# Two chained MLPs: a new order of three engines at the handover, and seven relayed waits in place of 21

## The chip, the core and the metric

The kernel runs on one core of a Trainium2 chip. The metric is the device time of a run in microseconds (us), the median of several runs. The engines that matter are TensorE (PE, matrix products), ScalarE (ACT) and VectorE (DVE), which read the products' results from PSUM and prepare the next operands in SBUF; GpSimd (POOL) does almost nothing, and SyncE (SP) issues the transfers. Each engine works through its own list of instructions strictly in the order in which the kernel's author wrote it. Semaphores are the only tie between the lists: an instruction waits until a count is reached, and everything behind it on its engine waits too.

## The reference

```
# q, k, v: 6016 tokens x 256 channels
qn, kn = q / norm over tokens, k / norm over tokens
a  = softmax(kn^T qn / tau)            # 256 x 256, over the channels
x1 = v @ a                             # 6016 x 256
h1 = x1 @ moe_w_in                     # 256 -> 2048
x2 = (h1 * cos(h1)) @ moe_w_out        # 2048 -> 256     first MLP
h2 = x2 @ moe2_w_in                    # 256 -> 2048
y  = (h2 * sigmoid(h2)) @ moe2_w_out   # 2048 -> 256     second MLP
```

## The kernel before

The first 60 us compute the softmax, which is then folded into the first MLP's input weights. After that come two passes over the tokens, one for each MLP. Tokens are cut into 12 tiles (`TILES`), tile 0 of 384 tokens and eleven of 512; a tile is worked on in halves of 192 or 256 columns. The 2048 hidden channels are cut into 4 steps a tile (`STEPS`). A step q therefore stands for one tile and one quarter of the hidden channels: steps 0 to 47 are the first MLP, steps 48 (`M1`) to 95 the second. Step 48 begins with tile 0 again, so the steps 48 to 51 are 192 columns wide.

A step's 2x2 block product is done in seven products in place of eight (a Strassen-Winograd form), with sums formed on ACT and DVE. Every number is split into a high and a low part, so each block takes three matmuls ("three passes"). In the code:

- `hidden(i, q)` is product i of the input side of step q, six matmuls (`xf_hi,h1w` in the first MLP, `xf_hi,h2w` in the second). It needs results of ACT and DVE: product 1 needs the PSUM bank pair of step q-2 free (`g_ps_ready`, `sil_ps_ready`), 6 and 2 need `s1`, 7 needs `s2`, 4 needs `s3`, 5 needs `c12` of step q-1, 3 needs `c22`.
- `output1(q, groups)` is the output side of the first MLP: eight groups of six matmuls (`g_hi,w1out`), always eight, of which group 0 waits for `lo_of_g(q)`.
- `output2(q, products)` is the output side of the second MLP: seven products (`g_hi,o2w`). Products 1, 2, 3 wait for `lo_s`, 5 and 7 for `lo_13`, 6 and 4 for `lo_24`. At step 48, products 5 and 6 also write PSUM banks that hold the first MLP's last result until ACT has moved it out (`move_x`, semaphore `x_moved`).
- On ACT (lines 469 to 594), `s1`, `s2`, `s3` copy products; `sine` and `hi_of_g` belong to the first MLP, `silu`, `silu_ps`, `hi_s`, `hi_13`, `hi_24` to the second; `hi_of_form(t)` splits the input of tile t.
- On DVE (lines 878 to 972), `c22`, `c12` form sums that `hidden` waits for; `gate`, `gate_ps`, `lo_of_g` belong to the first MLP; `t13`, `t2`, `t4`, `lo_s`, `lo_13`, `lo_24` to the second.

Inside an MLP the order within a step is always the same (`first_mlp(q)`, `second_mlp(q)`), and output runs three steps behind the hidden side in the first MLP (`output1(q - 3, ...)`) and two behind in the second. Around step 48 the order is written out by hand on each engine. There the first MLP's last three output steps (45, 46, 47) have to be worked off while the hidden side of steps 48, 49 and 50 begins.

A "relayed wait" sits in the middle of a product: `three_passes` issues its first matmul, and then the second one waits for `relay_done`, which POOL raises with a one-column memset (line 412) once `hidden(1, q)` is done. `RELAYED` (line 70) lists the steps q that have one. In the first MLP it stands in `output1(q - 3)`, group 1, in the second in `output2(q - 2)`, product 1; both come right behind `hidden(1, q)`. The data that the wait guards is not used by anyone: `relay` is read by nothing.

Of the kernel before, what the change touches and what calls it, by code (L numbers as in the profile page):

```python
# [27 lines left out]
def channel_attention_two_mlps(nc: bass.Bass, qk, v_tiles, tau, w_in1, w_out1, w_forms2, y_tiles):  # L28
# [21 lines left out]
    TILES = len(N)  # L50
    assert 2 * sum(N) == n_tokens and max(N) <= HALF
    STEPS = FC // 4
    M1 = TILES * STEPS
    ALL = 2 * M1
    LAST = ALL + 2

    def width(q):
        return N[q // STEPS % TILES]
# [8 lines left out]
        return 0 <= q < ALL  # L67


    RELAYED = [t * STEPS + 2 for t in range(2 * TILES) if t % TILES >= 1 + (t < TILES)]  # L70
    RELAY_TURN = {q: turn + 1 for turn, q in enumerate(RELAYED)}

    WP = 1024
# [10 lines left out]
    with ExitStack() as ctx:  # L84
# [203 lines left out]
        with nc.Block() as block:  # L288
# [126 lines left out]
            def _(act):  # L415
# [53 lines left out]
                def s1(q):  # L469
                    n = width(q)  # L470
                    act.wait_ge(p_done[1], q + 1)
                    if q < 2:
                        act.wait_ge(wu_slot7, q + 1)
                    if in1(q - 2):
                        act.wait_ge(g_ps_ready, q - 1)
                    if in2(q - 1):
                        act.wait_ge(sil_ps_ready, q - M1)
                    nc.scalar.activation(banks[:, c11_bank(q), :, 0:n], banks[:, c21_bank(q), :, 0:n],  # L478
                                         ACT.Copy).then_inc(s1_ready, 1)

                def s2(q):
                    n = width(q)
                    act.wait_ge(p_done[6], q + 1)
                    if q >= 1:
                        act.wait_ge(c12_ready, q)
                    nc.scalar.activation(s_part[:, 0, :, 0:n], banks[:, c21_bank(q), :, 0:n], ACT.Copy).then_inc(s2_ready, 1)  # L486

                def s3(q):
                    n = width(q)
                    act.wait_ge(p_done[7], q + 1)  # L490
                    if q >= 1:
                        act.wait_ge(c22_ready, q)
                    nc.scalar.activation(s_part[:, 1, :, 0:n], banks[:, c21_bank(q), :, 0:n], ACT.Copy).then_inc(s3_ready, 1)
# [30 lines left out]
                def hi_of_g(q):  # L524
                    n, b = width(q), q % 2
                    act.wait_ge(g_ready, q + 1)
                    act.wait_ge(g_ps_ready, q + 1)
                    if q >= 2:
                        act.wait_ge(out_done[1], q - 1)
                    else:  # L530
                        act.wait_ge(fold_ready, 2 * STEPS)
                    nc.scalar.activation(g_hi[:, 4 * b:4 * b + 4, :, 0:n], work[:, 4 * b:4 * b + 4, :, 0:n],
                                         ACT.Copy).then_inc(g_hi_ready, 1)

                def move_x(t, d):
                    n = N[t]
                    act.wait_ge(out_done[d], STEPS * (t + 1))
                    if t > 0:
                        act.wait_ge(x_stored, 16 * t)
                    nc.scalar.activation(xo[:, 2 * d:2 * d + 2, 0:n], banks[:, x_bank(t, d), :, 0:n],  # L540
                                         ACT.Copy, scale=TWO_PI).then_inc(x_moved, 1)

                def silu(q):
                    n, i = width(q), q - M1
                    act.wait_ge(c22_ready, q + 1)
                    act.wait_ge(c12_ready, q + 1)
                    if i > 0:
                        act.wait_ge(lo_s_ready, i)
                        act.wait_ge(t2_ready, i)
                    else:  # L550
                        act.wait_ge(g_lo_ready, M1 - 1)
                    nc.scalar.activation(work[:, 0:4:3, :, 0:n], h[:, q % 2, :, :, 0:n], ACT.Silu).then_inc(sil_ready, 1)  # L552

                def silu_ps(q):
                    n, i = width(q), q - M1
                    act.wait_ge(p_done[2], q + 1)
                    act.wait_ge(p_done[4], q + 1)
                    if i > 0:
                        act.wait_ge(lo_s_ready, i)
                        act.wait_ge(t4_ready, i)  # L560
                    else:
                        act.wait_ge(g_lo_ready, M1 - 1)
                    nc.scalar.activation(work[:, 1:3, :, 0:n], banks[:, q % 2:q % 2 + 2, :, 0:n],
                                         ACT.Silu).then_inc(sil_ps_ready, 1)
# [12 lines left out]
                def hi_13(q):  # L577
                    n, i = width(q), q - M1
                    act.wait_ge(t13_ready, i + 1)
                    if i > 0:  # L580
                        for o in (5, 7):
                            act.wait_ge(o_done[o], i)
                    else:
                        act.wait_ge(out_done[1], M1)
                    nc.scalar.activation(g_hi[:, 3:5, :, 0:n], work[:, 4:6, :, 0:n], ACT.Copy).then_inc(hi_13_ready, 1)
# [154 lines left out]
                sine(M1 - 1)  # L740
                silu_ps(M1)
                s1(M1 + 1)
                silu(M1)
                hi_of_g(M1 - 1)
                hi_s(M1)
                hi_of_form(TILES + 1)
                s2(M1 + 1)
                s3(M1 + 1)
                silu_ps(M1 + 1)
                s1(M1 + 2)  # L750
                hi_13(M1)
                hi_24(M1)
                silu(M1 + 1)
                s2(M1 + 2)
                hi_s(M1 + 1)
                move_x(TILES - 1, 0)
                move_x(TILES - 1, 1)
                hi_13(M1 + 1)
                s3(M1 + 2)
                for q in range(M1 + 3, LAST + 1):  # L760
# [3 lines left out]
            def _(dve):  # L764
# [453 lines left out]
                sums_of_form(TILES + 1)  # L1218
                phase(M1 - 1)
                lo_of_g(M1 - 2)  # L1220
                c22(M1)
                gate_ps(M1 - 1)
                c12(M1)
                gate(M1 - 1)
                lo_of_g(M1 - 1)
                t13(M1)
                lo_s(M1)
                t2(M1)
                c22(M1 + 1)
                t4(M1)  # L1230
                for q in range(M1 + 2, LAST + 1):
                    second_mlp(q)

# [1 line left out]
            def _(pe):  # L1235
# [284 lines left out]
                hidden(6, M1)  # L1520
                hidden(2, M1)
                hidden(5, M1)
                hidden(7, M1)
                output1(M1 - 3, (3, 4))
                hidden(4, M1)
                output1(M1 - 3, (5, 6, 7))
                hidden(3, M1)
                output1(M1 - 2, (0,))
                hidden(1, M1 + 1)
                output1(M1 - 2, (1, 2, 3, 4, 5, 6, 7))  # L1530
                hidden(6, M1 + 1)
                hidden(2, M1 + 1)
                hidden(5, M1 + 1)
                hidden(7, M1 + 1)
                hidden(4, M1 + 1)
                output1(M1 - 1, range(8))
                for q in range(M1 + 2, LAST):
                    second_mlp(q)


# [34 lines left out]
```

## Time and profile before

| | |
|---|---|
| median of 3 runs | 1046.9 us (1046.73 to 1046.99) |
| the profiled execution's own time | 1043.53 us |
| its span, first to last instruction | 1041.6 us |
| granted TensorE clock, mean | 0.997 |
| PE busy | 1019.6 us (98%) |
| DVE busy | 954.4 us (92%) |
| ACT busy | 806.4 us (77%) |

The span is 1.9 us shorter than the profiled execution's time, and that time is 3.4 us below the median of the runs that weren't profiled. A matmul's recorded duration is longer than the distance to the next one, since they are pipelined: what a matmul costs is the distance between two starts. A count (x...) in a view by windows also takes in the two or so matmuls that were still running when the window began.

### The profile page before, as it was taken

Reading aid. Unit: us, or ns where it says so; the run is one execution under the profiler, and the core shown is the slowest. Engines: PE = TensorE matmul, PEld = TensorE weight load, DVE = VectorE, ACT = ScalarE, POOL = GpSimd, SP = SyncE. Lnnn points to the kernel's source line nnn. Section 1 sums busy time; section 2 is a strip of 40 time slices with the busy share of each in tenths; the row PEclk is TensorE's granted clock in tenths of the full one; section 3 lists DMA queues with packets and bytes.
Section 4 is the critical chain, followed back from the end, with each engine's and each line's share of the span. In section 5 each row is a group of like instructions: output and inputs, shape, how many; then the busy total and the mean of one; then the engine's idle time right before and its main releaser. Section 6 shows DMA issues by size and latency. Waiting matters only on the chain. (4 is left out here: it accounts for less than half of the span.)

```text
span 1041.6 us, 21201 instructions
## 1 busy us (share of the span) xinstructions
PE 1019.6 (98%) x8718; PEld 1013.5 (97%) x8718; DVE 954.4 (92%) x1061; ACT 806.4 (77%) x875; POOL 2.9 (0%) x28
## 2 busy tenths in 40 slices
PE   7989999999999999999999899999999999999997
PEld 7979999999999999999999899999999999999997
DVE  7999989999999999998887389999999999999997
ACT  7779868788788788787777468877877878788775
POOL 0000000000000000000000000000000000000000
PEclk9999999999999999999999899999999999999999
DMA  8830110330331312304147211001001101101000
GB/s 286 289 97 6 36 37 21 112 132 21 112 112 42 112 68 82 116 22 163 36 162 274 100 42 37 4 38 42 20 23 42 41 2 42 42 2 41 22 22 21
DMA packets 18285, 76.03 MB, mean 73 GB/s; under 512 B 1808, under 2 KB 5904, under 8 KB 16144
## 3 DMA queue, kind: packets, MB, share of 16 engines
q1 hardware_dynamic: 18192, 74.72, 20.5%
q8 instruction: 67, 1.10, 0.4%
q14 instruction: 26, 0.21, 0.1%
HBM read 47.71 MB, written 27.00 MB: 72 GB/s over the span
## 5 line engine op out<-in xcount | busy, mean ns | idle before, releaser
L1241 PE MATMUL banks<-g_lo,w1out 128*128 128x256 f32 (+1 forms) x768 | 213.2, 278 | 0.0
L1242 PE MATMUL banks<-g_hi,w1out 128*128 128x256 f32 (+1 forms) x768 | 212.9, 277 | 0.0
L1238 PE MATMUL banks<-g_hi,w1out 128*128 128x256 f32 (+1 forms) x768 | 212.9, 277 | 0.0
L1238 PE MATMUL banks<-g_hi,o2w 128*128 128x256 f32 (+1 forms) x672 | 185.9, 277 | 3.8 <-ACT xo L540 1.5
L1238 PE MATMUL banks<-xf_hi,h1w 128*128 128x256 f32 (+1 forms) x672 | 186.8, 278 | 2.9 <-ACT banks L478 2.0
L1238 PE MATMUL banks<-xf_hi,h2w 128*128 128x256 f32 (+1 forms) x672 | 186.4, 277 | 1.9 <-ACT s_part L486 1.3
L1242 PE MATMUL banks<-xf_hi,h2w 128*128 128x256 f32 (+1 forms) x672 | 186.2, 277 | 0.0
L1241 PE MATMUL banks<-xf_lo,h2w 128*128 128x256 f32 (+1 forms) x672 | 186.2, 277 | 0.0
L1241 PE MATMUL banks<-g_lo,o2w 128*128 128x256 f32 (+1 forms) x672 | 185.9, 277 | 0.0
L1241 PE MATMUL banks<-xf_lo,h1w 128*128 128x256 f32 (+1 forms) x672 | 185.8, 276 | 0.0
L1242 PE MATMUL banks<-xf_hi,h1w 128*128 128x256 f32 (+1 forms) x672 | 185.8, 276 | 0.0
L1242 PE MATMUL banks<-g_hi,o2w 128*128 128x256 f32 (+1 forms) x672 | 185.7, 276 | 0.0
L1241 PEld LDWEIGHTS banks<-g_lo,w1out 128*128 128x128 f32 x768 | 145.3, 189 | 0.0
L1238 PEld LDWEIGHTS banks<-g_hi,w1out 128*128 128x128 f32 x768 | 145.1, 189 | 0.0
L1242 PEld LDWEIGHTS banks<-g_hi,w1out 128*128 128x128 f32 x768 | 145.1, 189 | 0.0
L1238 PEld LDWEIGHTS banks<-g_hi,o2w 128*128 128x128 f32 x672 | 126.6, 188 | 4.5 <-issue 1.7
L1238 PEld LDWEIGHTS banks<-xf_hi,h1w 128*128 128x128 f32 x672 | 126.4, 188 | 4.3 <-ACT banks L478 2.6
L1238 PEld LDWEIGHTS banks<-xf_hi,h2w 128*128 128x128 f32 x672 | 127.0, 189 | 2.2 <-ACT s_part L486 1.5
L1241 PEld LDWEIGHTS banks<-xf_lo,h2w 128*128 128x128 f32 x672 | 127.1, 189 | 0.0
L1242 PEld LDWEIGHTS banks<-xf_hi,h2w 128*128 128x128 f32 x672 | 127.1, 189 | 0.0
L1241 PEld LDWEIGHTS banks<-xf_lo,h1w 128*128 128x128 f32 x672 | 126.7, 188 | 0.1
L1242 PEld LDWEIGHTS banks<-g_hi,o2w 128*128 128x128 f32 x672 | 126.5, 188 | 0.0
(123 smaller groups left out, 2322.0 us busy)
## 6 DMA issues: line engine op xcount, KB each, us to landing
w_scr<-w_split SPq DMA_DIRECT2D x8, 1792.0 KB, 7.5
qk_raw<-qk SPq DMA_DIRECT2D x23, 512.0 KB, 4.5
h2w<-w_scr SPq DMA_DIRECT2D x4, 1792.0 KB, 8.0
o2w<-w_scr SPq DMA_DIRECT2D x4, 1792.0 KB, 8.1
form<-v_tiles SPq DMA_DIRECT2D x11, 512.0 KB, 3.5
x_scr<-xo SPq DMA_DIRECT2D x11, 512.0 KB, 2.6
form<-x_scr SPq DMA_DIRECT2D x11, 512.0 KB, 4.1
y_tiles<-xo SPq DMA_DIRECT2D x11, 512.0 KB, 5.0
```

The lines of the kernel that those rows point to most:

```text
L1238: nc.tensor.matmul(out, w_hi, m_hi, start=start, stop=False, skip_group_check=True)
L1241: nc.tensor.matmul(out, w_hi, m_lo, start=False, stop=False, skip_group_check=True)
L1242: return nc.tensor.matmul(out, w_lo, m_hi, start=False, stop=stop, skip_group_check=True)
```

## The change

Nothing is added to or taken from what is computed. Two things differ.

First, the order of the hand-written handover. PE lists the same products in another order, and now writes step 50 out by hand as well. ACT and DVE swap neighbours. On SyncE the list is the same.

Second, `RELAYED` holds 7 steps in place of 21. Before: step 2 of every tile from tile 2 on in the first MLP (q = 10, 14, ... 46) and from tile 1 on in the second (q = 54, 58, ... 94). Now: q = 7, 10, 14, 22 in the first MLP and q = 54, 58, 66 in the second.

```diff
-    RELAYED = [t * STEPS + 2 for t in range(2 * TILES) if t % TILES >= 1 + (t < TILES)]
+    RELAYED = [STEPS + 3] + [t * STEPS + 2 for t in (2, 3, 5, TILES + 1, TILES + 2, TILES + 4)]
...
@@ scalar engine @@
                 s1(M1 + 1)
+                hi_of_g(M1 - 1)
                 silu(M1)
-                hi_of_g(M1 - 1)
+                s2(M1 + 1)
+                s3(M1 + 1)
                 hi_s(M1)
                 hi_of_form(TILES + 1)
-                s2(M1 + 1)
-                s3(M1 + 1)
                 silu_ps(M1 + 1)
+                hi_13(M1)
                 s1(M1 + 2)
-                hi_13(M1)
+                move_x(TILES - 1, 0)
                 hi_24(M1)
                 silu(M1 + 1)
+                move_x(TILES - 1, 1)
                 s2(M1 + 2)
                 hi_s(M1 + 1)
-                move_x(TILES - 1, 0)
-                move_x(TILES - 1, 1)
@@ vector engine @@
+                gate_ps(M1 - 1)
                 c22(M1)
-                gate_ps(M1 - 1)
+                gate(M1 - 1)
                 c12(M1)
-                gate(M1 - 1)
                 lo_of_g(M1 - 1)
                 t13(M1)
+                t2(M1)
                 lo_s(M1)
-                t2(M1)
+                t4(M1)
                 c22(M1 + 1)
-                t4(M1)
@@ tensor engine @@
                 hidden(5, M1)
+                output1(M1 - 3, (3,))
                 hidden(7, M1)
-                output1(M1 - 3, (3, 4))
+                output1(M1 - 3, (4, 5))
                 hidden(4, M1)
-                output1(M1 - 3, (5, 6, 7))
+                output1(M1 - 3, (6, 7))
+                output1(M1 - 2, (0, 1))
+                hidden(1, M1 + 1)
+                output1(M1 - 2, (2,))
                 hidden(3, M1)
-                output1(M1 - 2, (0,))
-                hidden(1, M1 + 1)
-                output1(M1 - 2, (1, 2, 3, 4, 5, 6, 7))
+                output1(M1 - 2, (3,))
                 hidden(6, M1 + 1)
+                output1(M1 - 2, (4, 5, 6))
+                hidden(7, M1 + 1)
+                hidden(5, M1 + 1)
                 hidden(2, M1 + 1)
-                hidden(5, M1 + 1)
-                hidden(7, M1 + 1)
+                output1(M1 - 2, (7,))
+                output1(M1 - 1, (0,))
                 hidden(4, M1 + 1)
-                output1(M1 - 1, range(8))
-                for q in range(M1 + 2, LAST):
+                output1(M1 - 1, (1, 2, 3, 4, 5, 6, 7))
+                hidden(1, M1 + 2)
+                output2(M1, (3,))
+                hidden(3, M1 + 1)
+                output2(M1, (1,))
+                hidden(6, M1 + 2)
+                output2(M1, (2, 7))
+                hidden(5, M1 + 2)
+                output2(M1, (5, 4))
+                hidden(7, M1 + 2)
+                output2(M1, (6,))
+                hidden(2, M1 + 2)
+                hidden(4, M1 + 2)
+                for q in range(M1 + 3, LAST):
                     second_mlp(q)
```

ACT's list in the first half of the handover, before the change. L478 is `s1`, L552 `silu`, L532 `hi_of_g`, L575 `hi_s`, L438 `hi_of_form`, L486 `s2`, L493 `s3`, L563 `silu_ps`; the names in brackets are semaphores that the instruction waits for.

```order
L478 ACTIVATE banks<-banks 128x2x192 [waits sil_ps_ready,g_ps_ready,p1_done]
L552 ACTIVATE work<-h 128x2x2x192 [waits g_lo_ready,c12_ready,c22_ready]
L532 ACTIVATE g_hi<-work 128x2048 [waits out_done_1,g_ps_ready,g_ready]
L575 ACTIVATE g_hi<-work 128x6x192 [waits out_done_1,sil_ps_ready,sil_ready]
L438 ACTIVATE xf_hi<-form 128x1792 [waits p3_done,form_sum]
L486 ACTIVATE s_part<-banks 128x2x192 [waits c12_ready,p6_done]
L493 ACTIVATE s_part<-banks 128x2x192 [waits c22_ready,p7_done]
L563 ACTIVATE work<-banks 128x4x192 [waits lo_s_ready,t4_ready,p4_done,p2_done]
```

The same stretch now:

```order
L478 ACTIVATE banks<-banks 128x2x192 [waits sil_ps_ready,g_ps_ready,p1_done]
L532 ACTIVATE g_hi<-work 128x2048 [waits out_done_1,g_ps_ready,g_ready]
L552 ACTIVATE work<-h 128x2x2x192 [waits g_lo_ready,c12_ready,c22_ready]
L486 ACTIVATE s_part<-banks 128x2x192 [waits c12_ready,p6_done]
L493 ACTIVATE s_part<-banks 128x2x192 [waits c22_ready,p7_done]
L575 ACTIVATE g_hi<-work 128x6x192 [waits out_done_1,sil_ps_ready,sil_ready]
L438 ACTIVATE xf_hi<-form 128x1792 [waits p3_done,form_sum]
L563 ACTIVATE work<-banks 128x4x192 [waits lo_s_ready,t4_ready,p4_done,p2_done]
```

`s2` and `s3` of step 49 have moved ahead of `hi_s(48)` and `hi_of_form(13)`, and `hi_of_g(47)` ahead of `silu(48)`.

ACT's list in the second half, from `s1(50)` to `hi_13(49)`, before the change. L585 is `hi_13`, L594 `hi_24`, L540 `move_x`.

```order
L478 ACTIVATE banks<-banks 128x2x192 [waits sil_ps_ready,p1_done]
L585 ACTIVATE g_hi<-work 128x4x192 [waits out_done_1,t13_ready]
L594 ACTIVATE g_hi<-work 128x4x192 [waits t4_ready,t2_ready]
L552 ACTIVATE work<-h 128x2x2x192 [waits lo_s_ready,t2_ready,c12_ready,c22_ready]
L486 ACTIVATE s_part<-banks 128x2x192 [waits c12_ready,p6_done]
L575 ACTIVATE g_hi<-work 128x6x192 [waits o2_done,o1_done,o3_done,sil_ps_ready,sil_ready]
L540 ACTIVATE xo<-banks 128x512 [waits x_stored,out_done_0]
L540 ACTIVATE xo<-banks 128x512 [waits x_stored,out_done_1]
L585 ACTIVATE g_hi<-work 128x4x192 [waits o7_done,o5_done,t13_ready]
```

And now:

```order
L585 ACTIVATE g_hi<-work 128x4x192 [waits out_done_1,t13_ready]
L478 ACTIVATE banks<-banks 128x2x192 [waits sil_ps_ready,p1_done]
L540 ACTIVATE xo<-banks 128x512 [waits x_stored,out_done_0]
L594 ACTIVATE g_hi<-work 128x4x192 [waits t4_ready,t2_ready]
L552 ACTIVATE work<-h 128x2x2x192 [waits lo_s_ready,t2_ready,c12_ready,c22_ready]
L540 ACTIVATE xo<-banks 128x512 [waits x_stored,out_done_1]
L486 ACTIVATE s_part<-banks 128x2x192 [waits c12_ready,p6_done]
L575 ACTIVATE g_hi<-work 128x6x192 [waits o2_done,o1_done,o3_done,sil_ps_ready,sil_ready]
L585 ACTIVATE g_hi<-work 128x4x192 [waits o7_done,o5_done,t13_ready]
```

`hi_13(48)` has moved ahead of `s1(50)`, and the two `move_x` ahead of `hi_24(48)` and `s2(50)`.

## Rows read from the trace of the kernel before

**Rows 1.** The page, busy time of each engine.

```profile
PE 1019.6 (98%) x8718; PEld 1013.5 (97%) x8718; DVE 954.4 (92%) x1061; ACT 806.4 (77%) x875; POOL 2.9 (0%) x28
```

**Rows 2.** Windows: stretch, length, busy us (count) of each engine, granted clock, DMA.

```profile
556.58:595.24 38.66, 34.25 (x266) 33.60 (x265) 19.64 (x21) 19.55 (x23) 0.00 (x0) 0.91 0.51 201
573.80:577.20 3.40, 3.40 (x18) 3.40 (x18) 0.69 (x2) 0.81 (x1) 0.00 (x0) 0.50 0.25 105
590.90:594.20 3.30, 3.30 (x18) 3.30 (x17) 1.14 (x3) 0.95 (x2) 0.00 (x0) 0.50 0.02 5
595.30:605.90 10.60, 10.60 (x97) 10.60 (x97) 7.86 (x9) 6.80 (x10) 0.00 (x0) 1.00 0.31 100
133.50:165.30 31.80, 31.80 (x273) 31.80 (x272) 27.42 (x29) 23.64 (x23) 0.00 (x0) 1.00 0.10 30
165.50:206.00 40.50, 40.50 (x359) 40.50 (x358) 38.72 (x38) 32.89 (x32) 0.00 (x0) 1.00 0.24 85
288.00:550.00 262.00, 262.00 (x2311) 262.00 (x2311) 244.40 (x226) 210.18 (x206) 0.62 (x7) 1.00 0.25 91
740.00:1007.00 267.00, 267.00 (x2355) 267.00 (x2355) 256.15 (x306) 213.08 (x239) 0.69 (x7) 1.00 0.09 27
```

**Rows 3.** Timeline of PE, handover: start, duration, instruction, [idle before <- releaser].

```profile
571.94 0.36 PE L1238 MATMUL banks<-xf_hi,h2w 128*128 128x192 f32 x1 [1.32 <-ACT s_part L486]
...
573.43 0.36 PE L1238 MATMUL banks<-xf_hi,h2w 128*128 128x192 f32 x1 [0.58 <-ACT s_part L493]
...
585.74 0.36 PE L1238 MATMUL banks<-g_hi,o2w 128*128 128x192 f32 x1 [0.97 <-DVE g_lo L965]
...
589.54 0.33 PE L1238 MATMUL banks<-g_hi,o2w 128*128 128x192 f32 x1 [1.54 <-ACT xo L540]
```

**Rows 4.** Timeline of ACT, handover.

```profile
557.99 1.92 ACT L521 ACTIVATE work<-work 128x2048 f32<-128x2048 f32 x1
560.16 1.28 ACT L563 ACT_TABLE_LOAD   x1 [0.24 <-DVE g_lo L927]
561.45 0.81 ACT L563 ACTIVATE work<-banks 128x768 f32<-128x768 f32 x1
...
564.09 0.84 ACT L552 ACTIVATE work<-h 128x768 f32<-128x768 f32 x1
564.83 1.91 ACT L532 ACTIVATE g_hi<-work 128x2048 fp32r<-128x2048 f32 x1
568.76 1.17 ACT L575 ACTIVATE g_hi<-work 128x1152 fp32r<-128x1152 f32 x1 [2.03 <-PE banks L1242]
569.83 1.68 ACT L438 ACTIVATE xf_hi<-form 128x1792 fp32r<-128x1792 f32 x1
571.41 0.47 ACT L486 ACTIVATE s_part<-banks 128x384 f32<-128x384 f32 x1
572.89 0.49 ACT L493 ACTIVATE s_part<-banks 128x384 f32<-128x384 f32 x1 [1.00 <-PE banks L1242]
...
583.47 0.47 ACT L478 ACTIVATE banks<-banks 128x384 f32<-128x384 f32 x1 [7.86 <-PE banks L1242]
583.86 0.84 ACT L585 ACTIVATE g_hi<-work 128x768 fp32r<-128x768 f32 x1
...
588.80 1.08 ACT L540 ACTIVATE xo<-banks 128x512 f32<-128x512 f32 x2
```

**Rows 5.** Timeline of DVE, handover.

```profile
560.44 1.21 DVE L921 TENSOR_TENSOR work<-work,banks 128x1024 f32<-128x1024 f32 x1
...
584.72 0.96 DVE L965 TENSOR_TENSOR g_lo<-work,g_hi 128x768 fp32r<-128x768 f32 x1 [10.23 <-ACT g_hi L585]
```

**Rows 6.** Timeline of POOL: the first relay memset.

```profile
165.40 0.10 POOL L412 MEMSET relay<- 128x1 f32 x1 [163.94 <-PE banks L1242]
```

**Rows 7.** Timeline of PE at the second relayed wait.

```profile
206.48 0.31 PE L1241 MATMUL banks<-g_lo,w1out 128*128 128x256 f32 x1
206.62 0.28 PE L1242 MATMUL banks<-g_hi,w1out 128*128 128x256 f32 x1
```

## The prediction

> **What bounds the kernel now.** I read the page first. PE is busy for 98% of the span, DVE for 92%, ACT for 77% [rows 1]. So two questions are left: where does PE stand still, and how far apart do its matmuls start where it doesn't? The view of waits and the timeline of PE answer the first. Between the start-up and the last output step, which the change doesn't touch, PE has one cluster of stalls, in the handover. There are four, each with its releaser [rows 3]:
>
> - 571.94, product 7 of step 49, released by `s2(49)`. ACT started `s2` at 571.41 because `hi_s(48)` and `hi_of_form(13)` stood ahead of it [rows 4]; its own input, product 6, had ended near 569.1 (PE ran dry near 570.5, two products of 0.67 us later).
> - 573.43, product 4 of step 49, released by `s3(49)`: product 4 stood right behind product 7, and `s3` (0.49 us) had no room between them.
> - 585.74, output product 7 of step 48, released by `lo_13(48)` on DVE, which had idled 10.23 us for `hi_13(48)` [rows 5]. That was queued on ACT behind `s1(50)`, which waited 7.86 us for PE [rows 4].
> - 589.54, output product 5 of step 48, released by the first `move_x` at 588.80, which was queued behind `hi_s(49)`.
>
> The view by windows shows that the granted clock fell to 0.50, that is 1.2 of 2.4 GHz, in two stretches, each just behind two such stalls (from 573.80 and from 590.90) [rows 2]. Elsewhere in the handover it was 1.00.
>
> The same view answers the second question. Leaving out the matmuls still running at a window's start, about 2.4, the 256-column ones start 31.80/270.6 = 0.1175 us apart from 133.5 to 165.3, and 40.50/356.5 = 0.1136 us apart from 165.5 to 206 [rows 2]. It is the same code at two paces, at full clock in both. What lies between is the first relayed wait [rows 6]. The faster pace then holds: 262/2308.5 = 0.1135 from 288 to 550, and 267/2352.5 = 0.1135 from 740 to 1007. So a relayed wait puts PE into the quicker pace, and once there it stays. Why, the trace doesn't show.
>
> **Part 1, the handover.** Both kernels hold the same products between 556.58 (behind hidden product 5 of step 48) and the end of product 4 of step 50, at 595.24 before. That is 38.66 us with 266 - 2 = 264 matmuls: 21 output groups of the first MLP, 126 matmuls of 256 columns, and 138 of 192. Without stalls and at full clock, at the slower pace, which the change doesn't alter here, they take 126 x 0.1175 = 14.8 us, plus 138 x 10.60/94.6 = 0.112, 15.5 us (the window from 595.30) [rows 2]. Together 30.3 us, so 8.4 us can go. The other way round: four idle times of 1.32 + 0.58 + 0.97 + 1.54 = 4.41 us, each 0.16 us short of what it costs (a 0.27 us matmul's successor starts after 0.11), make 5.05 us. The low clock costs 3.40 - 16 x 0.1135 = 1.6 and 3.30 - 16 x 0.112 = 1.5 us. That is 8.2 us, with the edges of the slow stretches left out. I take 8.4.
>
> Whether it goes depends on what is late next. I laid the new lists side by side, with 0.67 us for a product of 192 columns, 0.705 for a group of 256, and the durations of rows 4 and 5. A PE result is usable some 0.16 us after its product's slot ends. "Ready" is when the operand is there, "wanted" when PE reaches the product:
>
> - `gate_ps(47)` for product 1 of step 49: product 7 of step 48 now ends at 557.96, so `s3(48)` ends 558.6, `sine(47)` (1.92) at 560.5, `gate_ps` (1.21, now first on DVE) at 561.7. Wanted 562.9.
> - `s1(49)` for product 6: product 1 ends 563.5, ready 564.2, wanted 565.6.
> - `s2(49)` for product 7: ACT does `hi_of_g(47)` 564.1 to 566.0, `silu(48)` to 566.7 (its `c12(48)` is there at 565.7), `s2` to 567.1. Wanted 568.4.
> - `s3(49)` for product 4: product 7 ends 569.1, ready 569.7, wanted 571.8. Three products and two groups stand between now.
> - `lo_s(48)` for output product 3: output step 46 ends 571.1, `hi_s` (1.17) 572.4, `lo_s` about 573.8, wanted 578.1.
> - `lo_13(48)`: output step 47 ends 577.4, `hi_13` 577.6 to 578.4, `lo_13` (0.96) to 579.4, wanted 581.4.
> - `s1(50)`, now behind `hi_13`: ready 578.8, wanted 580.1.
> - both `move_x`: ready about 579.4 and 581.5, wanted 582.8 and 584.8.
> - `s2(50)`: ready 582.0, wanted 584.1. `s3(50)`, behind `hi_s(49)` and `hi_13(49)`: product 7 ends 584.8, ready 585.4, wanted 586.2. This is the tightest, 0.8 us, and is the spacing that `second_mlp` has in every step.
>
> What the moves delay: `hi_s(48)` and `hi_of_form(13)` (1.68 us) run 3 to 4 us later on ACT's clock, and behind them stands `silu_ps(49)`, done by 575.2 and needed for `s1(50)` at 578. DVE's `c12(48)` waits for product 3 of step 48 until 565.0, with only `lo_of_g(47)` queued behind it, which ends at 568.3 and is wanted at 571.1. SP's list is the same; its weight load for step 50 waits for the end of output step 46 and starts 2.6 us later, some 20 us before that step's output. ACT's table load (1.28 us) stays one load, ahead of `silu_ps(48)`. I charge nothing for any of these: the slack above covers them. If one cover fails it costs what is short, bounded above by the longest stall of before, 1.7 us, and 1.7 more if the clock falls; below nothing, since no product becomes shorter.
>
> **Part 2, the earlier relayed wait.** A step of the first MLP is 90 matmuls. The wait at q = 7 stands three steps ahead of the one at q = 10, that is 3 x 90 x 0.1175 = 31.7 us before 165.4, at 133.7. From there everything is 256 columns wide. If it does what the one at 165.4 did, 270 matmuls gain 0.1175 - 0.1135 = 0.004 us each: 1.1 us. Bounds: nothing, if the pace doesn't turn there (the wait at q = 10 is still in the list), and 1.2 by the step lengths. At the quicker pace DVE must keep up: it is busy for 38.72 of 40.50 us in the following tile, where weight work comes on top, and PE has no stall there; here it has 27.42 of 31.80 [rows 2]. So no charge. I take 1.1, since the one example seen, in the same place of a step, worked.
>
> **Part 3, 14 relayed waits fewer.** In the quick pace such a wait costs the distance 206.62 - 206.48 = 0.14 less 0.1135 [rows 7]: 0.03 us. 14 fewer give 0.4 us. Bounds: 0 and 0.5. What goes with them is the insurance. From q = 22 to the handover, 260 us, and from q = 66 to the end, some 290 us, nothing resets the pace. Against a slip speaks that in the windows of 262 and 267 us, waits every 40 us never found a slow pace to repair: the mean 0.1135 leaves no room for even one slow tile.
>
> The TensorE page of the Trainium skill (TensorE: Matmul & The Clock Gate, "Back-to-back issue gap") gives an isolated full-clock gap of N/2.4 + 2.5 ns, which is 109 ns at 256 columns as an estimate, and knows no second pace. By it the wait at q = 7 would bring nothing, which is rival 1 below, and the sum would be 8.8 us. The trace differs: 0.1175 and 0.1135 us at full clock.
>
> **Sum.** 8.4 + 1.1 + 0.4 = 9.9 us. The profiled execution's 1043.5 us becomes 1033.6. It stands 3.4 us below the median of the runs, and nothing here depends on that difference, so 1046.9 - 9.9 = 1037.0 us.
>
> **Rivals.**
>
> 1. *The wait at q = 7 doesn't turn the pace.* Only one turn is seen after a slow stretch of the first MLP, so a turn may need a position that happens to fit. Then 1.1 us are missing, the extra wait costs 0.03: 1038.1 us.
> 2. *A new wait takes the place of an old one in the handover.* My lists are hand-timed to a few tenths, and the slack is 0.8 to 1.4 us at five places. A stall of about 1 us costs 1 us, and with a second one close by the clock falls again (1.7): 1038.0 to 1039.7 us. Against it: the two pairs of stalls before came from waits of 2 us and more.
> 3. *The clock falls without the stalls,* for instance from the change of widths. Then 3.3 us stay: 1040.3 us. Against it: both falls stand right behind two stalls, and none elsewhere.
> 4. *Slower: the pace slips where no relayed wait is left.* At 0.1175 a matmul, an unguarded stretch loses 3.5%, 9 us from q = 22 on and 10 from q = 66 on. Eating up the 9.9 us takes 280 of the 550 unguarded us, that is a slip at the beginning of one stretch and an early one in the other. Both at once: 1037.0 + 19 = 1056 us. For it speaks that a slow pace did come about by itself: the stretch from 133.5 on follows the narrow tile 0. Against it: after 165 us no slip anywhere in uniform work.
>
> **How the numbers follow.** The forecast has a chance of 62%, rival 1 of 13%, rival 2 of 13%, rival 3 of 4%. A slip as in rival 4 has 8%, of which 3 end slower than before. The forecast's own range is 1036.2 to 1037.8 (the remainders of the terms: +-0.4 on the handover, 0.1 on each of the others, 0.2 between sessions). To hold 8 in 10 it has to take in rivals 1 and 2: 1036.1 to 1039.7. About 0.2% is what a measurement can tell here; faster by more than that 0.95, within it 0.02, slower 0.03.
>
> **What the profile would show.** Right: no PE idle time over 0.3 us between 550 and 590, granted clock 1.00 there, product 4 of step 50 ending near 586.9 - 1.1 - 0.2 = 585.6; `s2(49)` ahead of `hi_s(48)` on ACT; POOL memsets at about 133.7 and then 164.3, with 0.1135 us between matmuls in between; 0.1135 from 290 to 540 and from 730 to the end; PE's total gap 9.9 us smaller. Wrong: a memset at 133.7 with 0.1175 behind it (rival 1), a wait on `s3`, `s1` or `lo_13` in the handover (rival 2), a window at 0.50 (rival 3), or 0.1175 anywhere behind q = 22 outside the narrow tile (rival 4).

## The result, and the profile after

The changed kernel took 1034.86 us (median of 4 runs, 1033.86 to 1036.12) beside 1046.82 us for the kernel before (4 runs, 1046.03 to 1046.99). That is 12.0 us less, a ratio of 0.9888 with a 95% interval of 0.9871 to 0.9905. The predicted 1037.0 us was 2.1 us too high, and its range, from 1036.1, missed the median. The two profiled executions differ by less: 1043.53 and 1034.61 us, 8.9 us. The start-up (up to the first full-width `hidden` product) takes 1.6 us off that difference: it ends at 103.5 us in the trace before and at 105.0 in this one, although both kernels are the same up to there.

Page part 1 of the kernel after; it answers [rows 1].

```profile
span 1032.7 us, 21187 instructions
PE 1015.8 (98%) x8718; PEld 1010.7 (98%) x8718; DVE 954.4 (92%) x1061; ACT 806.6 (78%) x875; POOL 1.5 (0%) x14
```

The same windows, where they have a counterpart [rows 2]: the handover, the stretch between the memsets of q = 7 and q = 10, and one long stretch without a relayed wait in each MLP.

```profile
556.00:586.00 30.00, 30.00 (x267) 30.00 (x267) 19.37 (x22) 20.30 (x24) 0.00 (x0) 1.00 0.67 268
135.30:165.70 30.40, 30.40 (x270) 30.40 (x269) 27.09 (x29) 23.52 (x23) 0.00 (x0) 1.00 0.11 32
290.00:550.00 260.00, 260.00 (x2296) 260.00 (x2296) 242.53 (x223) 208.62 (x204) 0.00 (x0) 1.00 0.25 92
732.00:1000.00 268.00, 268.00 (x2367) 268.00 (x2366) 257.12 (x310) 214.33 (x240) 0.00 (x0) 1.00 0.09 27
```

PE is busy through the whole handover, at a granted clock of 1.00; before, 34.25 of 38.66 us at 0.91. Less the 2.4 matmuls that were running at a window's start, the other three windows give 0.1136, 0.1134 and 0.1133 us a matmul: the quick pace begins at q = 7, and it holds for 260 and 268 us without a wait.

The timeline of ACT in the handover, whose rows answer [rows 4].

```profile
558.66 1.91 ACT L521 ACTIVATE work<-work 128x2048 f32<-128x2048 f32 x1
...
566.68 0.48 ACT L486 ACTIVATE s_part<-banks 128x384 f32<-128x384 f32 x1
569.26 0.49 ACT L493 ACTIVATE s_part<-banks 128x384 f32<-128x384 f32 x1 [2.10 <-PE banks L1242]
571.41 1.17 ACT L575 ACTIVATE g_hi<-work 128x1152 fp32r<-128x1152 f32 x1 [1.66 <-PE banks L1242]
572.48 1.69 ACT L438 ACTIVATE xf_hi<-form 128x1792 fp32r<-128x1792 f32 x1
...
577.53 0.84 ACT L585 ACTIVATE g_hi<-work 128x768 fp32r<-128x768 f32 x1 [2.16 <-PE banks L1242]
578.28 0.47 ACT L478 ACTIVATE banks<-banks 128x384 f32<-128x384 f32 x1
578.69 0.58 ACT L540 ACTIVATE xo<-banks 128x512 f32<-128x512 f32 x1
...
584.82 0.49 ACT L493 ACTIVATE s_part<-banks 128x384 f32<-128x384 f32 x1 [0.45 <-PE banks L1242]
```

`s2(49)` ends at 567.2 (forecast 567.1), `s3(49)` at 569.8 (569.7), `hi_13(48)` at 578.4 (578.4), `s3(50)` at 585.3 (585.4). The times can be compared as they stand, since both traces reach step 48 at almost the same time (552.53 and 552.65 us): the longer start-up happens to cancel what was gained behind q = 7. On DVE, `lo_13(48)` follows at once, and DVE idles 3.50 us ahead of it where it idled 10.23 [rows 5]:

```profile
578.40 0.96 DVE L965 TENSOR_TENSOR g_lo<-work,g_hi 128x768 fp32r<-128x768 f32 x1 [3.50 <-ACT g_hi L585]
```

### The profile page after: what moved, and what is told of

Same layout as the page of the kernel before. It is cut to its first block, busy times and chain, and to the rows that moved or that the text cites. A ratio compares the mean times of both kernels' runs of the same rounds, so it can differ in the third digit from the quotient of the medians.

```text
span 1032.7 us, 21187 instructions
## 1 busy us (share of the span) xinstructions
PE 1015.8 (98%) x8718; PEld 1010.7 (98%) x8718; DVE 954.4 (92%) x1061; ACT 806.6 (78%) x875; POOL 1.5 (0%) x14
## 4 chain that ended last, share of the span: by engine, by line
PE 96%; DVE 1%; ACT 1%; issue 1%; DMA 0%; DVEq 0%; ACTq 0%
PE banks L1238 31%; PE banks L1241 30%; PE banks L1242 30%; PE banks L1254 2%; PE banks L1256 2%; PE banks L1258 1%; PE banks L1264 0%; DMA qk_raw<-qk 0%; ACT w1in_hi L431 0%; ACT g_hi L575 0%; ACT work L521 0%; DVE wr L856 0%; DVE qk_lo L767 0%; DVE h L893 0%; DVE g_lo L965 0%
## 5 line engine op out<-in xcount | busy, mean ns | idle before, releaser
L1238 PEld LDWEIGHTS banks<-xf_hi,h1w 128*128 128x128 f32 x672 | 127.2, 189 | 4.2 <-ACT banks L478 2.6
L1242 PEld LDWEIGHTS banks<-xf_hi,h1w 128*128 128x128 f32 x672 | 127.1, 189 | 0.0
L1242 PEld LDWEIGHTS banks<-xf_hi,h2w 128*128 128x128 f32 x672 | 126.4, 188 | 0.0
```

The costliest lines, as they stand in the source:

```text
L1238: nc.tensor.matmul(out, w_hi, m_hi, start=start, stop=False, skip_group_check=True)
L1242: return nc.tensor.matmul(out, w_lo, m_hi, start=False, stop=stop, skip_group_check=True)
```

## The experiments

All times are medians, and each group is compared with runs of the kernel before on its own chip.

**The kernel before, six traces.** The first question was what the first trace had less of than the first median. Five more executions of the unchanged file were traced.

> The kernel before, word for word, for a second trace and for the spread of its runs. Its trace behind the prediction was an execution of 1043.5 us, 3.4 us below the median of its other runs. Theory A (the missing 2 us come from stretches at the lower granted clock that this one trace happened to have few of): this execution takes 1045 to 1047 us, and its trace shows more time at granted clock 0.50 than the 3.4 + 3.3 us of the first, in the handover or in the start-up between 60 and 90 us. Theory B (the pace of TensorE differs from run to run): the trace shows 0.1175 us between matmuls in uniform work somewhere behind 165 us. Theory C (an offset outside the span): span plus 1.9 us no longer gives the time.

> The kernel before once more, for a third trace. Theory B (whether a relayed wait turns the pace is chance): the spacing from 166 to 207 us is 0.1175 or 0.1135, and the segment between the first and the second memset is 42.4 or 40.8 us, nothing between. Theory A (the low clock varies): the segment from step 48 to the memset of step 54 is 72.0 us with one fall less, or 73.6 us. The time of this execution differs from the first trace's by the sum of such pieces and by the start-up's (103.4 to 105.8 us up to the first full-width product).

> The kernel before, a fourth trace, to find out what its executions above 1046 us hold. If the time comes out above 1045.8: the start-up up to the first full-width product takes 105 us or more (in place of 103.4 to 104.2), or the wait at q = 10 fails to turn the pace (segment 42.4 in place of 40.8 us), or both; the handover segment is 72.0 or 73.6 us. If it comes out below: the same pieces add up to less.

> The kernel before, a fifth trace, with the same expectation: the time is the sum of start-up (103.4 to 105.8 us), the segment up to q = 14 (with 1.6 us for each tile in which the wait failed) and the handover (72.0 or 73.6 us), within 0.2 us.

> The kernel before, a sixth trace, with the same expectation. Together the six say how often each piece occurs, and so whether the 3.4 us between the first trace and the first median can be made of them.

Measured, with segments read from the starts of PE and POOL instructions (us). "Start-up" ends where the first full-width `hidden` product starts; "tile 2" is the distance from the memset of q = 10 to that of q = 14; "handover" goes from step 48's first matmul to the memset of q = 54.

| trace | time | start-up | tile 2 | handover |
|---|---|---|---|---|
| before, first | 1043.5 | 103.5 | 40.8 | 73.6 |
| e1 | 1044.4 | 104.2 | 42.4 | 72.0 |
| e8 | 1044.3 | 104.0 | 40.8 | 73.7 |
| e10 | 1044.2 | 103.9 | 42.4 | 72.2 |
| e11 | 1046.6 | 106.5 | 42.4 | 72.0 |
| e12 | 1043.5 | 103.1 | 42.4 | 72.1 |
| after, first | 1034.6 | 105.0 | 40.8 | 64.9 |
| after, e4 | 1036.5 | 105.8 | 40.8 | 64.9 |
| after, e14 | 1035.7 | 105.0 | 40.8 | 64.9 |

Theory B's sign, the slow pace behind 165 us, is there in four of the five new traces. Theory A did not come as written: e1 took 1044.4 us, below its 1045, with as much time at the low clock as the first trace (one stretch of 3.4 us in the start-up and one in the handover, in place of two in the handover). But the low clock does vary in both places. What lies outside the span is 1.9 to 2.0 us in all (theory C is out). By the medians, e1 (1044.66 us, 10 runs, ratio 1.0003) and e8 (1044.48, 10 runs, 1.0001) are the same as before. The trace above 1046 us is e11. Its windows in the start-up, one inside the handover, and then the two tiles behind q = 10 and q = 14:

```profile
72.00:82.00 10.00, 9.53 (x54) 9.44 (x55) 7.06 (x14) 4.79 (x11) 0.00 (x0) 0.66 0.01 2
579.00:583.00 4.00, 4.00 (x23) 4.00 (x22) 0.09 (x1) 0.81 (x1) 0.00 (x0) 0.57 0.07 29
134.00:168.00 34.00, 34.00 (x291) 34.00 (x290) 29.31 (x31) 24.44 (x24) 0.00 (x0) 1.00 0.09 29
168.50:210.50 42.00, 42.00 (x359) 42.00 (x358) 38.77 (x38) 32.80 (x32) 0.00 (x0) 1.00 0.23 82
211.00:291.00 80.00, 80.00 (x708) 80.00 (x707) 76.55 (x73) 65.30 (x64) 0.10 (x1) 1.00 0.24 86
```

And its relay memsets:

```profile
168.35 0.10 POOL L412 MEMSET relay<- 128x1 f32 x1 [166.88 <-PE banks L1242]
210.76 0.10 POOL L412 MEMSET relay<- 128x1 f32 x1 [42.31 <-PE banks L1242]
251.60 0.10 POOL L412 MEMSET relay<- 128x1 f32 x1 [40.75 <-PE banks L1242]
```

At 168.35 the relayed wait did nothing: 42.00/356.6 = 0.1178 us a matmul for another tile. The next, at 210.76, turned the pace (80.00/705.6 = 0.1134). The granted clock was low in the start-up for some 30 matmuls in a row, 6.4 us, against some 15 in e1, e8 and e10 and none in the first trace and e12. So the start-up ends at 103.1 to 106.5 us, later than e11's own expectation allowed, and the changed kernel's varies as well (105.0 to 105.8). Over all 17 traces it ends at 103.1 to 103.5 us without low clock, at 103.6 to 105.0 with one such stretch of 15 matmuls and at 105.8 to 106.5 with two: the low clock goes with most of the spread, not with all of it. The handover holds one low stretch in four traces and two in the others. The trace of 1046.6 us is 3.06 us above the first: 3.01 from the start-up, 1.57 from tile 2, less 1.62 in the handover.

Over all these comparisons, 14 of 52 runs of before were above 1046 us (and 5 of 20 in e1 and e8), and its medians on four further chips were 1044.6 to 1045.3 us. The first median of 1046.9 us, on which the prediction was built, stands for 4 runs of 4 above 1046 us.

The traces show one more thing. Whether the first relayed wait turns the pace goes with something that happens some 9 us ahead of q = 7, in code that is the same in all the kernels here. Between two narrow output groups of tile 0 stand 24 full-width matmuls. Here are the first and the twenty-first of them, in the first trace of the kernel after (above) and in e4 (below):

```profile
125.92 0.30 PE L1238 MATMUL banks<-xf_hi,h1w 128*128 128x256 f32 x1
128.30 0.28 PE L1242 MATMUL banks<-xf_hi,h1w 128*128 128x256 f32 x1
```

```profile
126.68 0.30 PE L1238 MATMUL banks<-xf_hi,h1w 128*128 128x256 f32 x1
129.00 0.28 PE L1242 MATMUL banks<-xf_hi,h1w 128*128 128x256 f32 x1
```

The distance is 2.38 us in the one and 2.31 in the other, and in the 17 traces of this document it is always one of these two. Where it was 2.38, the first relayed wait turned the pace, 8 times of 8 (the first trace before, e8, e2, after, e3, e13, e9, e7; e6 has no wait). Where it was 2.31, the first wait did nothing, 8 times of 8 (e1, e10, e11, e12, e4, e14, e5, e15), and the second wait turned the pace every time. Before the wait, all 17 ran at the slow pace again. Why the two cases arise, and how they reach the wait, no run shows.

**The two halves of the change.** `RELAYED` of before in the file of after (e2), and of after in the file of before (e3), beside the changed kernel (e4).

```diff
# e2: after, with
+    RELAYED = [t * STEPS + 2 for t in range(2 * TILES) if t % TILES >= 1 + (t < TILES)]
# e3: before, with
+    RELAYED = [STEPS + 3] + [t * STEPS + 2 for t in (2, 3, 5, TILES + 1, TILES + 2, TILES + 4)]
```

> The new order of the handover with the 21 relayed waits of before. The prediction's own terms: 8.4 us faster than before. Theory A: 10 to 11 us faster, since the typical run of before loses more in the handover than its trace showed. Theory B: 8.4 to 9 us faster. In the trace no stall and no low clock between 550 and 590 us under all of them.

> The old order of the handover with the seven relayed waits of after. The prediction's own terms: 1.1 + 0.4 = 1.5 us faster than before. Theory A: the same 1.5 us, as the waits have nothing to do with the handover's stalls. Theory B: 3 to 4 us faster. The four stalls of the handover stay under all of them.

> The changed kernel again, beside the two halves: 11 to 12.5 us faster than before. If the two halves are independent, the gain of the order and the gain of the waits sum to this within 0.7 us. Its handover shows no low clock; what still varies between its runs lies in the start-up before 100 us (theory A).

Measured against 1044.82 us (19 runs, 1043.97 to 1047.91): the order alone 1035.87 (ratio 0.9919, 0.9902 to 0.9935), 9.0 us faster; the waits alone 1043.17 (0.998, 0.9968 to 0.9992), 1.7 us faster; both 1035.51 (0.9911, 0.9894 to 0.9927), 9.3 us faster, not 11 or more. The halves sum to 10.6, 1.3 us more than the whole and more than the 0.7 expected; the spread of single runs (e3: 1039.8 to 1045.5) leaves it open whether that is a difference. In e2's trace the handover has no stall and no low clock. In e3's all four stalls are there, as expected, with one low stretch, behind the first pair:

```profile
573.20:576.50 3.30, 3.30 (x18) 3.30 (x17) 0.03 (x1) 0.81 (x1) 0.00 (x0) 0.50 0.06 26
```

The stretch from 290 to 550 us in e2, with six waits, has three matmuls less than the kernel after in the same 260 us:

```profile
290.00:550.00 260.00, 260.00 (x2293) 260.00 (x2293) 242.32 (x224) 208.10 (x204) 0.59 (x6) 1.00 0.26 92
```

Three matmuls are 0.3 us, 0.05 us a wait.

**No waits, and a wait in every step.**

```diff
# e6: after, with
+    RELAYED = []
# e7: after, with
+    RELAYED = list(range(STEPS + 3, M1)) + list(range(M1 + STEPS + 2, ALL))
```

> The changed kernel without any relayed wait. If only such a wait turns TensorE to the quicker pace, all uniform work from 134 us on runs at 0.1175 us a matmul: 3450 matmuls up to the handover and 3600 behind it, each 0.004 us dearer, is 28 us, so 26 to 30 us slower than the changed kernel. Rival (the pace turns by itself sooner or later, as in the narrow tile of the handover): less than 10 us slower. Rival (the waits only cost): 0.3 us faster than the changed kernel.

> The changed kernel with a relayed wait in every step, 83 in place of 7. At the 0.03 us of the prediction the 76 more cost 2.3 us; at the 0.045 us that the segments of the traces with 21 and 7 waits show, 3.4 us. Against this stands a turn to the quick pace at step 8 or 9 at the latest where q = 7 misses it, worth up to 1.2 us. So 1.5 to 3.5 us slower than the changed kernel. In the trace the spacing is 0.1135 plus one longer distance a step.

Without waits 1049.84 us (three runs of 4 at 1049.7 to 1050.0, one at 1066.0); before on the same chip 1044.59. The changed kernel didn't run on that chip; by its times and gains on the others this is 14 to 15 us slower than it, half of what was expected, except in one run. The windows of the trace say why:

```profile
135.00:165.00 30.00, 30.00 (x257) 30.00 (x256) 25.59 (x27) 22.73 (x22) 0.00 (x0) 1.00 0.11 32
290.00:550.00 260.00, 260.00 (x2210) 260.00 (x2209) 235.12 (x218) 199.94 (x196) 0.00 (x0) 1.00 0.24 86
640.00:1000.00 360.00, 360.00 (x3179) 360.00 (x3178) 346.48 (x412) 288.38 (x322) 0.00 (x0) 1.00 0.09 29
```

The whole first MLP ran at 260/2207.6 = 0.1178 us, and behind the narrow tile of the handover the second MLP ran at 0.1133 with no wait at all. In this trace the pace changed across the narrow tile of the handover, and uniform work kept what it had. The run of 1066 us would be one with the slow pace in both MLPs: 3600 matmuls at 0.0044 us more are 16 us (it took 16.2 us more than the median), and its granted clock, 0.998, was no lower than that of the others. It was not traced, so this is not shown.

A wait in every step: 1037.36 us, ratio 0.994 (0.9923 to 0.9957). Its memsets in the first MLP:

```profile
143.70 0.10 POOL L412 MEMSET relay<- 128x1 f32 x1 [10.15 <-PE banks L1242]
153.95 0.10 POOL L412 MEMSET relay<- 128x1 f32 x1 [10.15 <-PE banks L1242]
```

A step is 10.25 us with its wait, so four steps are 41.0 us. A tile with one wait is 40.84 us, so three more waits add 0.16, again 0.05 us each. The kernel is 7.2 us faster than before on its chip, 2 to 3 us less than the changed kernel is on the others, within the 1.5 to 3.5 expected.

**Which list does the work.** e5 keeps the new lists of ACT and DVE and the seven waits, and puts back TensorE's old handover. e13 keeps TensorE's new handover and puts back the second half of ACT's list.

```diff
# e5: after, TensorE's hand-written steps from hidden(5, M1) on as in before
# e13: after, scalar engine
-                hi_13(M1)
                 s1(M1 + 2)
-                move_x(TILES - 1, 0)
+                hi_13(M1)
                 hi_24(M1)
                 silu(M1 + 1)
-                move_x(TILES - 1, 1)
                 s2(M1 + 2)
                 hi_s(M1 + 1)
+                move_x(TILES - 1, 0)
+                move_x(TILES - 1, 1)
```

> The new lists of ScalarE and VectorE and the seven waits, but TensorE's handover in the order of before. If the stalls came from what stood ahead of s2(49), hi_13(48) and move_x on ScalarE, three of the four stalls go with these lists alone, and only the wait of product 4 of step 49 for s3(49) stays (0.74 us beyond the pace), because product 7 stands right ahead of it. A single short stall: if the clock falls only after two stalls close together, it stays at 1.00 and the kernel is 0.7 to 1 us behind the changed one. Rival: one stall is enough for a clock fall, then 2.3 to 2.6 us behind. Rival: TensorE's own order is what cures them, then 5 us or more behind.

> The changed kernel with ScalarE's second half as before: hi_13(48) behind s1(50), both move_x behind hi_s(49). TensorE's new order puts three more products between output step 47 and output product 7 of step 48, so lo_13 should still be in time (ready 580.6, wanted 581.4). move_x would now wait for hi_s(49), which waits for output product 2: ready near 583.7, wanted 582.8. So one stall of about 1 us at output product 5, a granted clock of 1.00, and 0.8 to 1.3 us slower than the changed kernel. Rival: the clock falls too, 2.4 to 3 us slower. Rival: the moves in this half weren't needed, the same time.

e5: 1036.71 us against 1044.59, ratio 0.9932 (0.9915 to 0.9948), 7.9 us faster. Three of the four stalls are gone, and the one that stays is the expected one, a wait for `s3(49)`; the window over the handover has no low clock.

```profile
572.21 0.36 PE L1238 MATMUL banks<-xf_hi,h2w 128*128 128x192 f32 x1 [0.58 <-ACT s_part L493]
```

```profile
560.00:600.00 40.00, 39.35 (x344) 38.98 (x343) 25.18 (x31) 23.67 (x31) 0.00 (x0) 1.00 0.49 184
```

Its handover segment is 66.3 us against 64.9 with TensorE's new order and 72.0 to 73.7 before. So of the 7.1 to 8.8 us that the handover gives, ACT's and DVE's lists alone bring all but 1.4, where 0.7 to 1 was expected. The stall is 0.74 of that. The trace has the rest in two pieces. A shorter hold-up, which shows as only 0.07 us of idle time, stands ahead of this matmul, which starts 0.35 us behind the one before it:

```profile
561.71 0.36 PE L1238 MATMUL banks<-xf_hi,h2w 128*128 128x192 f32 x1
```

With the slower matmuls beside it, it costs about 0.35 us. And the two long runs of full-width output groups go at the slow pace (42 matmuls from 563.84 at 0.1184 us and 48 from 572.97 at 0.1182), where the changed kernel takes 0.1146 for the 42 from 572.46: 90 x 0.0037, about 0.33 us.

The reverse, TensorE's new order with ACT's whole old list, was not tried: `s2(49)` would stand behind `hi_s(48)`, which waits for output step 46 (group 7), which TensorE's new order puts behind product 7 of step 49, which waits for `s2(49)`, so it would deadlock.

e13: 1035.65 us, ratio 0.9909 (0.9887 to 0.9931), beside 1034.73 for the changed kernel on the same chip. One stall, for `move_x`, and none for `lo_13`, as expected; no low clock.

```profile
583.03 0.33 PE L1238 MATMUL banks<-g_hi,o2w 128*128 128x192 f32 x1 [1.02 <-ACT xo L540]
```

```profile
560.00:600.00 40.00, 38.98 (x347) 38.84 (x346) 26.06 (x32) 24.52 (x32) 0.00 (x0) 1.00 0.48 180
```

The segment is 66.1 us: 1.2 us for moving two copies forward. In these two traces single stalls of 0.74 and 1.2 us left the clock at 1.00, and each low stretch of before followed a pair of stalls within 4 us. That is no proof that a single stall is safe: of the 14 pairs in the seven traces with the old lists, 9 were followed by a low stretch and 5 were not, and each single stall was traced once.

**Waits close together, and many runs of both.**

```diff
# e9, e15: after, with
+    RELAYED = [STEPS + 3, STEPS + 4, STEPS + 5, STEPS + 6, M1 + 6, M1 + 7]
```

> The changed kernel with its waits drawn together: q = 7, 8, 9, 10 and 54, 55 in place of 7, 10, 14, 22, 54, 58, 66. The traces so far say that a wait turns a slow pace 3 times in 5 at q = 7 and 5 times in 6 at q = 10, and that a quick pace is never lost in uniform work. So the turn comes at q = 7 or one step (10.6 us, worth 0.4 us) later instead of three, which is 0.3 us in the mean, and one wait less gives 0.05: 0.2 to 0.5 us faster than the changed kernel, 9.3 to 10 us faster than before. Rival (a later wait is needed because the pace slips again or q = 7 to 10 can all fail): some executions 1.6 to 15 us slower than the changed kernel's.

> The changed kernel again, to have many runs of both kernels on one chip. If the prediction's terms are right and the rest was the draw of the start-up's clock: 9.0 to 10.2 us faster than before. If the change also takes away something that the traces haven't shown: 11 us or more. Its own runs spread from 1033.5 to 1036.5 us, by the start-up (0, 3.2 or 6.4 us at low clock) and by whether q = 7 turns the pace.

> The version with waits at q = 7, 8, 9, 10, 54, 55 on the same chip as the changed kernel: 0.2 to 0.5 us faster than it in the mean by the traces' pieces, which the spread of either (2.5 us) may hide.

e14, the changed kernel: 1034.73 us (6 runs, 1033.28 to 1036.02) against 1044.68 (11 runs, 1043.34 to 1048.34), 9.95 us faster, ratio 0.9897 (0.9880 to 0.9915). e15 beside it: 1034.71 us (5 runs, 1034.23 to 1035.07), the same; e9 on another chip: 1034.71 against 1045.29, ratio 0.990 (0.9880 to 0.9919), 10.6 us faster where 9.3 to 10 was expected. No execution fell behind, so the rival of a pace that slips again didn't show. In e9's trace q = 7 turned the pace; e15's memsets show what happens where q = 7 fails:

```profile
134.46 0.10 POOL L412 MEMSET relay<- 128x1 f32 x1 [132.99 <-PE banks L1242]
145.07 0.10 POOL L412 MEMSET relay<- 128x1 f32 x1 [10.51 <-PE banks L1242]
155.32 0.10 POOL L412 MEMSET relay<- 128x1 f32 x1 [10.15 <-PE banks L1242]
```

One step at the slow pace (10.61 us), then 10.25: the wait at q = 8 caught it. In e14's trace q = 7 failed too, and the wait at q = 10 came only after three slow steps. By the median, the close waits gain nothing that can be measured.

## Why the prediction was wrong

The sum of the change was right and the number it was taken from was not. The step that failed is the last of the sum: "It stands 3.4 us below the median of the runs, and nothing here depends on that difference, so 1046.9 - 9.9 = 1037.0 us." The runs show in its place that 1046.9 us does not stand for the kernel before: its medians on four other chips, with 9 to 19 runs each, were 1044.6 to 1045.3 us, only 1.1 to 1.8 us above the traced execution and not 3.4. There the gain is 9.3 (e4) and 9.95 us (e14) where 9.9 was predicted, and the changed kernel took 1035.5 and 1034.7 us, about the 1034.9 of the first comparison. So it was the median of before that stood out there, by about 2 us, and the forecast with it.

What separates one execution from another is made of pieces that either kernel can have: up to 3.4 us of start-up, more of it where the clock is low there; 1.6 us for the tile in which a relayed wait fails; and, before, 1.6 us for a second low stretch in the handover. Why all four runs of the first comparison lay above 1046 us stays open. At the 14 of 52 found on the other chips, four of four would come up by chance about once in 200 times (an estimate, (14/52) to the fourth), so something in that chip or that session is a rival that no run tested. e11 shows what one run above 1046 us holds, and none above 1047 us was traced.

The gain came out right partly by luck. In the mean of the traces (six of before, three of after, start-up left out) the handover gives 72.6 - 64.9 = 7.7 us where 8.4 was forecast, and everything outside it, that is the two terms of the relayed waits, 2.2 where 1.5 was forecast. The two errors, 0.7 us each, cancel.

Point by point:

- *The handover, 8.4 us.* 73.58 - 64.90 = 8.7 us between the first two traces, no stall, clock 1.00: right. But 73.6 was the costlier of two cases. Four of six traces of before have one low stretch there and lose 7.1 to 7.3 us. The prediction took one trace's two stretches as fixed.
- *The hand-timed lists.* Right to 0.1 us at four places, and e5 and e13 put back single stalls at the place and about the size forecast before them (0.74 and 1.2 us). Rival 2, a new wait in the handover, did not come.
- *The earlier wait, 1.1 us.* Rival 1 was held to be another case; it occurs from one execution to the next. q = 7 turned the pace in 5 of 9 traces; where it did, the three steps took 30.6 us in place of 31.8, 1.2 us less. And the wait at q = 10 of before, taken as sure, failed in 4 of 6, which costs the kernel before 1.57 us each time and is part of why this term was too small. "I take 1.1, since the one example seen, in the same place of a step, worked" rests on one trace of one of the two cases shown above.
- *14 waits fewer, 0.4 us.* A wait costs 0.05, not 0.03 us: 0.7 us. The prediction took only the one distance at the wait, rounded to 0.01 us. The distances just behind it are wider as well: 0.144, 0.120, 0.120, 0.118 and 0.118 us at the third wait of the first trace, 0.053 us in all beyond the pace of 0.1133 (0.04 at the second wait, which the prediction read).
- *Rival 4, a slip.* None: 0.1134 and 0.1133 us a matmul over both windows, and in no trace behind the turn of the pace. *Rival 3*, a low clock without stalls: none in the handover of the ten traces with the new lists or a part of them, eight of them without a stall.
- *The Trainium skill's formula.* By the Trainium skill (TensorE: Matmul & The Clock Gate, "Back-to-back issue gap"), the isolated gap at full clock is N/2.4 + 2.5 ns, an estimated 109 ns at 256 columns, and no second pace is named, so the waits would be worthless. The traces have two, 0.1134 and 0.1178 us, and e6 puts the waits at 14 to 15 us.

## What to carry to other kernels

Before taking a forecast gain from a median, ask what separates the profiled execution from that median; with one trace and three runs the range has to hold it on both sides. In a handover between two steady loops, look at what stands ahead of each small copy that TensorE needs: on ScalarE, moving two copies ahead of work that nobody waited for was worth 1.2 us, and the ScalarE and VectorE lists together most of the gain. A stall costs its idle time and 0.16 us, and two close together can cost 1.6 us more of low clock. And one trace of a kernel shows one of several cases: a wait that worked in it failed in four of the next five.

## What the runs showed of the hardware

- Back-to-back matmuls of 256 columns, each with its own weight load, ran at two stable paces at full clock, 0.1178 and 0.1134 us. Uniform work kept the one it had, for 436 us in e6 (slow, from 131.6 to 567.8 us) and 360 us (quick). Across the narrow tile of the handover the pace changed by itself in e6.
- A wait in the middle of a product, some 0.05 us long, turned slow to quick in 16 of 24 cases (5 of 9 at q = 7, 1 of 1 at q = 8, 6 of 10 at q = 10, 4 of 4 at q = 14), and was never seen to turn quick to slow. The eight failures are the first waits of the eight traces with the distance of 2.31 us above; no first wait failed in the others, and no second wait failed at all.
- The granted clock in the start-up was low for 0, 15 or 30 matmuls in different executions of the same program. In the six traces of before, the wait at q = 10 failed exactly where the handover then had one low stretch in place of two, so that 1.57 and 1.55 us nearly cancel. A failed wait isn't needed for that: in e3 the wait at q = 7 turned the pace, and the handover had one low stretch as well. Nor is it the same stretch each time: it followed the first pair of stalls in e11 and e3, the second in e1, e10 and e12. What decides between the two is open.
